# One fp32 mLSTM + MLP + four-expert kernel: GpSimd's order of weight pieces, and who prepares the input blocks of the second token half

## The reference, cut to what matters

```python
def _attn_ref(q, k, v, i_gate, f_gate, o_gate):   # (2, 8, 768, 40): a stabilized linear recurrence
    for t in range(S):
        C = f_stab * C + i_stab * outer(v_t, k_t);  n = f_stab * n + i_stab * k_t
        y_t = sigmoid(o_t) * (C q_t) / max(|n q_t|, 1)

def _moe_ref(x, w_in, w_out):                     # d_ff = 2048: "layer one" below
    h = x @ w_in
    return (h - np.tanh(h)) @ w_out

def _moe2_ref(x, domain_probs, w1, w2):           # 4 experts, 1024 hidden: "the experts" below
    p = domain_probs / (domain_probs.sum(-1, keepdims=True) + 1e-09)
    for e in range(4):
        out += p[:, e:e+1] * (np.maximum(x @ w1[e], 0.0) @ w2[e])
```

## Time and profile before

| what | us |
|---|---|
| median of 3 runs | 582.3 (580.66 to 582.67) |
| the profiled execution's own time | 584.62 |
| its span in the trace | 582.8 |
| PE busy | 567.1 (97%) |
| DVE, ACT, POOL busy | 346.7, 246.1, 245.3 |
| mean granted clock of TensorE | 0.991 of full speed |

### The profile page before, as it was taken

The page is one execution under the profiler, slowest core; times in us unless marked ns, Lnnn a source line. Parts: engine busy times, 40 slices in busy tenths (PEclk is TensorE's granted clock), DMA queues, the critical chain, the costliest instruction groups (busy, mean ns, idle before and its releaser), DMA issues.

```text
span 582.8 us, 10092 instructions
## 1 busy us (share of the span) xinstructions
PE 567.1 (97%) x3796; PEld 544.7 (93%) x3796; DVE 346.7 (59%) x663; ACT 246.1 (42%) x501; POOL 245.3 (42%) x238
## 2 busy tenths in 40 slices
PE   9999999999999999979999998999998999999997
PEld 8989999999998877869999998999998999999997
DVE  6656556555554486568754755645844646764644
ACT  5775645565534554524234432234522235422221
POOL 4878423333202677574006665026663046650000
PEclk9998999999999999989999999999998999999999
DMA  7977445654235021060002111002122002100201
GB/s 275 346 260 243 141 123 160 170 169 105 52 71 148 5 58 58 2 164 8 2 1 58 60 60 60 1 1 60 58 60 60 1 15 58 48 0 1 69 1 69
DMA packets 46359, 48.08 MB, mean 83 GB/s; under 512 B 21830, under 2 KB 36422, under 8 KB 46310
## 3 DMA queue, kind: packets, MB, share of 16 engines
q1 hardware_dynamic: 46208, 47.39, 27.2%
q10 hardware_dynamic: 102, 0.05, 0.0%
HBM read 41.12 MB, written 4.73 MB: 79 GB/s over the span
## 4 chain that ended last, share of the span: by engine, by line
PE 72%; POOL 11%; DMA 7%; DVE 3%; SPq 2%; issue 2%; ACT 1%; DVEq 0%; POOLq 0%; ACTq 0%
PE bank L1712 6%; PE bank L1713 6%; PE bank L1714 6%; DMA fast_raw<-in_w 5%; PE bank L1687 5%; PE bank L1690 5%; PE bank L1688 5%; PE bank L1689 5%; PE bank L1669 4%; PE bank L1670 3%; PE bank L1671 3%; PE bank L1640 3%; PE bank L1642 3%; PE bank L1641 3%; POOL fast_w L837 3%; POOL fast_w L829 2%
## 5 line engine op out<-in xcount | busy, mean ns | idle before, releaser
L1359 DVE TENSOR_TENSOR x<-bank,x 128x384 f32<-128x384 f32 x160 | 88.8, 555 | 75.6 <-PE bank L1690 73.6
L1712 PE MATMUL bank<-fast_w,g_tiles 128*128 128x320 f32 x384 | 119.8, 312 | 0.0
L1713 PE MATMUL bank<-fast_w,g_tiles 128*128 128x320 f32 x384 | 119.2, 310 | 0.0
L1714 PE MATMUL bank<-fast_w,g_tiles 128*128 128x320 f32 x384 | 119.1, 310 | 0.0
L1036 ACT ACTIVATE g_tiles<-x 128x384 fp32r<-128x384 f32 x96 | 50.4, 525 | 148.0 <-DVE x L1359 147.5
L1353 DVE SCALAR_TENSOR_TENSOR g_tiles<-x,g_tiles 128x384 fp32r<-128x384 f32 x96 | 69.7, 733 | 18.1 <-ACT g_tiles L1036 14.2
L1713 PEld LDWEIGHTS bank<-fast_w,g_tiles 128*128 128x128 f32 x384 | 73.1, 190 | 0.0
L1712 PEld LDWEIGHTS bank<-fast_w,g_tiles 128*128 128x128 f32 x384 | 72.9, 190 | 0.2 <-DVE arena L1301 0.2
L1714 PEld LDWEIGHTS bank<-fast_w,g_tiles 128*128 128x128 f32 x384 | 72.6, 189 | 0.0
L1306 DVE TENSOR_TENSOR bank<-bank,g_tmp 128x384 f32<-128x384 f32 (+2 forms) x64 | 36.1, 565 | 54.5 <-ACT g_tmp L991 54.1
L829 POOL TENSOR_TENSOR fast_w<-fast_raw,fast_w 128x512 fp32r<-128x512 f32 x16 | 21.7, 1356 | 96.0 <-ACT fast_w L977 95.9
(11 more groups left out here) (226 smaller groups left out, 1326.0 us busy)
## 6 DMA issues: line engine op xcount, KB each, us to landing
w_raw<-in_w SPq DMA_DIRECT2D x8, 704.0 KB, 7.3
zb<-z SPq DMA_DIRECT2D x10, 512.0 KB, 4.6
feat<-in_feat SPq DMA_DIRECT2D x10, 512.0 KB, 3.9
fast_raw<-in_w SPq DMA_DIRECT2D x16, 320.0 KB
tok<-in_tok SPq DMA_DIRECT2D x10, 484.0 KB, 4.6
fast_raw<-in_w SPq DMA_DIRECT2D x16, 256.0 KB
fast_raw<-in_w SPq DMA_DIRECT2D x32, 128.0 KB
spare<-xg SPq DMA_DIRECT2D x8, 256.0 KB, 2.8
```

The costliest lines, as they stand in the source:

```text
L1359: V.tensor_tensor(out, bank_of(u, name)[:, 0:WIDE], other, ALU.add).then_inc(summed, 1)
L1712: mm(out, g_tiles[:, k, 0, c], high_w, start=first, stop=False)
L1713: mm(out, g_tiles[:, k, 0, c], low_w, start=False, stop=False)
L1714: mm(out, g_tiles[:, k, 1, c], high_w, start=False, stop=stop).then_inc(third_done, 1)
```

## The change

1. Layer one's tables: `xa_low`, `xa_high`, `high_at` and `down_at` are shifted by a step in places; DVE casts a piece's second-layer weights before the low part of a block and not after it; ACT copies the first half of piece 3 in unit 0 of the experts and not in step 63.
2. POOL adds the x sums of the second half in two parts: the 256 main features before the tails have come, the tails after.
3. The blocks of the second half are made in later units (none in unit 1, five high parts in unit 2, two in unit 3), and POOL makes the low parts of T1 to T4; DVE keeps those of B11, B21 and B22. POOL does this ahead of the sums of piece 4. PE waits for each block apart.
4. For experts 1 to 3, POOL makes the low parts of pieces q and q+1 right behind each other, then the sums and the low parts of q+2, then those of q+3. Before, the sums of piece q+1 stood ahead of the low parts of piece q throughout. ACT copies the second-layer weights before the first-layer ones.

```diff
-        xa_high = {50: (B11,), 51: (B21,), 52: (B22,), 55: (T1, T2), 58: (T3, T4)}
-        xa_low = {53: B11, 54: B21, 55: B22, 56: T1, 57: T2, 59: T3, 60: T4}
-        high_at = {53: (0, 0), 54: (0, 1), 56: (1, 0), 57: (1, 1), 59: (2, 0), 60: (2, 1), 63: (3, 0)}
-        down_at = {54: 0, 56: 1, 60: 2, 62: 3}
+        xa_high = {50: (B11,), 51: (B21,), 52: (B22,), 55: (T1, T2), 59: (T3, T4)}
+        xa_low = {53: B11, 54: B21, 55: B22, 56: T1, 58: T2, 60: T3, 61: T4}
+        high_at = {53: (0, 0), 54: (0, 1), 57: (1, 0), 58: (1, 1), 60: (2, 0), 61: (2, 1)}
+        down_at = {53: 0, 57: 1, 60: 2, 63: 3}
...
+            def add_x_parts():
+                pool.wait_ge(x2_main, 8)
+                pool.wait_ge(block_ready, BLOCKS)
+                pool.wait_ge(xt_ready, len(L1_SIZES))
+                for i, one, two_ in x_parts(1):
+                    after(pool, x_main_sums, i - T1)
+                    G.tensor_tensor(x_sum(1, i)[:, 0, :], one[:, 0, :], two_[:, 0, :], ALU.subtract).then_inc(x_main_sums, 1)
+                pool.wait_ge(x_main_sums, 4)
+                pool.wait_ge(tails_in, 256)
+                for i, one, two_ in x_parts(1):
+                    after(pool, x_sums, 4 + i - T1)
+                    G.tensor_tensor(x_sum(1, i)[:, 1, :], one[:, 1, :], two_[:, 1, :], ALU.subtract).then_inc(x_sums, 1)
+
+            def x_block_low(i):
+                src, x = x_sum(1, i), x_block(1, i)
+                pool.wait_ge(block_high, BLOCKS + i + 1)
+                after(pool, late_ready, 2 * (i - T1))
+                G.tensor_tensor(x[:, 2, :], src[:, 0, :], x[:, 0, :].bitcast(F32), ALU.subtract).then_inc(late_ready, 1)
+                pool.wait_ge(late_ready, 2 * (i - T1) + 1)
+                G.tensor_tensor(x[64:KT, 1, :], src[64:KT, 1, :], x[64:KT, 1, :].bitcast(F32),
+                                ALU.subtract).then_inc(late_ready, 1)
...
-            add_x(1)
+            add_x_parts()
+            for i in (T1, T2, T3, T4):
+                x_block_low(i)
             pool.wait_ge(down_done, L1_STEPS)
-            add_weights(PPU)
-            for q in range(PPU, FAST):
-                if q + 1 < FAST:
-                    add_weights(q + 1)
+            for e in range(1, EXPERTS):
+                q = PPU * e
+                if e == 1:
+                    pool.wait_ge(late_ready, 8)
+                add_weights(q)
+                add_weights(q + 1)
                 low_weights(q)
+                low_weights(q + 1)
+                add_weights(q + 2)
+                low_weights(q + 2)
+                add_weights(q + 3)
+                low_weights(q + 3)
...
                 q = fast_at[u]
+                high_of_down(q)
                 high_weights(q, 0)
-                high_of_down(q)
...
                 if u == 0:
+                    high_weights(PPU - 1, 0)
                     evac(len(L1_SIZES) - 1)
...
-                if u == 2:
-                    x_block_high(1, B22)
-                if u == 3:
-                    x_block_high(1, T3)
+                for i in {2: (B11, B21), 3: (T3, T4)}.get(u, ()):
+                    x_block_high(1, i)
...
-                for i in {1: (B11, B21), 2: (T1, T2), 3: (T4,)}.get(u, ()):
-                    x_block_high(1, i)
+                if u == 2:
+                    for i in (B22, T1, T2):
+                        x_block_high(1, i)
...
-                if u in (1, 2, 3):
-                    x_block_low(1, {1: B11, 2: B22, 3: T3}[u])
+                if u == 3:
+                    x_block_low(1, B21)
```

More of the change, by code:

```diff
@@ L346, in mlstm_mlp_experts @@
         block_ready = sem("block_ready")
+        x_main_sums = sem("x_main_sums")
+        late_ready = sem("late_ready")
         fast_in = [sem(f"fast_in{r}") for r in range(FAST_RING)]
@@ L838, in low_weights, with x_parts @@
                                         w[:, F_DN:F_DN + 2 * D].bitcast(F32), ALU.subtract).then_inc(fast_down, 1)
[L840 to L850, removed]
+            def x_parts(h):
+                return ((T1, plain(h, -1), plain(h, B11)), (T2, plain(h, B22), x_sum(h, T1)),
+                        (T3, plain(h, B22), plain(h, -1)), (T4, plain(h, B21), x_sum(h, T2)))
@@ new lines, in add_x @@
+            def add_x():
+                pool.wait_ge(x2_main, 6)
+                pool.wait_ge(tails_in, 128)
+                for i, one, two_ in x_parts(0):
+                    after(pool, x_sums, i - T1)
+                    G.tensor_tensor(x_sum(0, i), one, two_, ALU.subtract).then_inc(x_sums, 1)
+            def add_x_parts():
[10 more added lines that the diff above has]
+                    G.tensor_tensor(x_sum(1, i)[:, 1, :], one[:, 1, :], two_[:, 1, :], ALU.subtract).then_inc(x_sums, 1)
@@ L852, in _ @@
             add_weights(0)
-            add_x(0)
+            add_x()
             for q in range(PPU):
@@ L1344, in _ @@
                     evac(m // L1_TILES - 1)
+                if m in down_at:
+                    high_of_down(down_at[m])
                 if m in xa_low:
                     x_block_low(0, xa_low[m])
-                if m in down_at:
-                    high_of_down(down_at[m])
             def low_tile(u, k, src):
@@ L1383, in _ @@
                     mix(v, TPH - 1)
-                if u in (2, 3, 4):
-                    x_block_low(1, {2: B21, 3: T2, 4: T4}[u])
                 low_tile(u, C11, bank_of(u, 2)[:, 0:WIDE])
@@ L1408, in _ @@
                 if u == 2:
-                    x_block_low(1, T1)
+                    x_block_low(1, B11)
+                if u == 3:
+                    x_block_low(1, B22)
             for tt in range(TPH):
@@ L1714, in third, with plain_block, sum_block @@
                 mm(out, g_tiles[:, k, 1, c], high_w, start=False, stop=stop).then_inc(third_done, 1)
-            def new_half(u, j):
-                if u % (2 * PPU) == PPU and u < 2 * PPU:
-                    pe.wait_ge(block_ready, BLOCKS + j + 1)
+            def plain_block(u, i):
+                if u == PPU:
+                    pe.wait_ge(block_ready, BLOCKS + i + 1)
+            def sum_block(u, i):
+                if u == PPU:
+                    pe.wait_ge(late_ready, 2 * (i - T1 + 1))
             for m in range(L1_STEPS):
@@ L1752, in _ @@
                     pe.wait_ge(fast_up, 2 * (4 * (u // (2 * PPU)) + u % PPU + 1))
-                new_half(u, B11)
+                plain_block(u, B11)
                 pe.wait_ge(summed, 5 * (u - 1) + (SUM_U2 if u == 1 else SUM_C21))
@@ L1757, in _ @@
                 third(u - 1, 1)
-                new_half(u, T2)
+                sum_block(u, T2)
                 if u > 1:
@@ L1764, in _ @@
                 third(u - 1, 3)
+                plain_block(u, B21)
                 pe.wait_ge(first_copied, u + 1)
@@ L1768, in _ @@
                 third(u - 1, 5)
-                new_half(u, T3)
+                sum_block(u, T3)
                 pe.wait_ge(summed, 5 * u + SUM_U2)
@@ L1777, in _ @@
                 third(u - 1, 9)
-                new_half(u, T4)
+                sum_block(u, T4)
                 pe.wait_ge(summed, 5 * u + SUM_U3)
@@ L1781, in _ @@
                 third(u - 1, 10)
+                plain_block(u, B22)
                 pe.wait_ge(summed, 5 * u + SUM_C22)
```

## The result

| | before | after |
|---|---|---|
| median of the runs of one session, us | 582.48 (580.66 to 584.56, 4 runs) | 574.01 (573.42 to 574.25, 4 runs) |
| ratio of the times, with its 95% interval | | 0.985 [0.982, 0.989] |
| the profiled execution, us | 584.62 | 573.42 |
| span, us; mean granted clock | 582.8; 0.991 | 571.6; 1.000 |
| PE busy, us | 567.1 (97%) | 563.1 (99%) |

The account below looks back on a forecast made before the run. PE was busy 567.1 of 582.8 us, so only its idle time and clock could be won. Terms 5.8 + 5.7 - 1.2 - 0.5 = 9.8 us off the median 582.3 gave 572.5 us; range 569 to 577.5.

Parts of the forecast that it names:

- Unit 1: Unit 1 of the experts: with no blocks there, PE's 4.1 us stop and 1.7 of clock go, 5.8 us off.
- half price for half an x sum: POOL's x sums, second half: half a sum takes half of 2.0, so 1.0 us; bounds 1.0 and 2.0.
- DVE's blocks in units 2 and 3: B11 at the end of unit 2 can collide with POOL's T3 and T4: 0 to 2.2 us, taken as 0.
- The two waits for POOL: PE's two 2.0 us waits for POOL's last low part of a piece go, with 1.7 of clock: 5.7 us.
- The new wait for C11: Units 9, 17 and 25: ACT's copy waits for POOL's sums and holds tile C11, 0.4 us each.
- with more room: Unit 9, on ACT: second high copy and tile C22 queue behind the late copy with more room; no cost added.
- The term "1.2": Units 9, 17 and 25: three waits of 0.4 us for tile C11, 1.2 us lost; bounds 0 and 2.4.
- Layer one: Layer one's waits for low parts: 2.7 us against 2.2, a loss of 0.5; bounds a gain of 1.6, a loss of 2.4.
- the 1 us that it gave as a sign: Layer one: waits of about 1 us after steps 53 and 60 would show the forecast holds.
- The 0.8 at step 57: Layer one, step 57: the wait from ACT, held by the sums of piece 1, goes, 0.8 us.
- The clock: PE's clock was to stand at 1.00 from 210 to 570 us; 1.7 us counted with each of two removed stalls.
- The rival in which the port takes the gain back: DVE loses at steps 53 and 60, C11 waits 0.8, one stall halves the clock: 5.0 us gained, 577.3; chance 0.15.

Follow-up runs that it names:

- part 4 alone: Kernel before plus only POOL's low parts of two pieces behind each other and ACT's second-layer copy first: 579.08 us, ratio 0.996.
- part 4 alone without ACT's swap: Kernel before plus only POOL's new order of pieces, ACT's first high copy still ahead of its second-layer copy: 576.56 us, ratio 0.991.
- part 1 alone: Kernel before plus only layer one's new tables, the cast ahead of the block and piece 3 copied in unit 0: 583.18 us, ratio 1.001.
- parts 2 and 3 alone: Kernel before plus only x sums in two parts, second-half blocks in later units and T1 to T4 low by POOL: 577.41 us, ratio 0.990.

## Why the prediction was right, point by point

- **Unit 1: right.** 5.8 forecast, 5.7 measured. From unit 1 to unit 5 the blocks alone give 5.1, as the whole change does. DVE's fifth sum waits for nothing but its product. The half price for half an x sum (1.0) was measured at 1.07 to 1.20.
- **DVE's blocks in units 2 and 3 at 0: off by 0.6**, inside the bounds of 0 to 2.2. B11 didn't collide, since POOL waited for T3's high part just then (row at 265.05). B21 in unit 3 did, with T4's low part, and unit 4 began 0.37 late; B22 did in unit 4, with the sums of piece 4 that now run there, and cost the other 0.20. That sums of weights would meet a block was in neither the term nor its bounds.
- **The two waits for POOL: right.** 5.7 forecast, 5.8 measured. Piece 7's low parts end at 337.9, PE begins unit 11 at 346.8: 8.9 us to spare, 7.5 forecast.
- **The new wait for C11: the mechanism right, the term too small.** Sums of piece 7 were forecast to end at 337.8 on the clock of before, and C11 to be ready at 339.95; measured, with 7.9 added, 337.8 and 340.0, and a wait of 0.40 in the list where 0.4 was forecast (0.56 by the starts). The step that failed is the sentence that the second high copy and tile C22 are queued behind it "with more room". I counted room for ACT, not the port: the late tile moved C22 behind the start of a POOL instruction. The term "1.2" measured 3.5 when its cause alone was taken away, and 3.2 against before, which had lost 0.3 in units 17 and 25 itself. Beside it stands 1.0 that nobody forecast: units 7, 15 and 23 and the ones next to them are 0.1 to 0.25 shorter than before. The net is the 2.2 of the table; part of the size of the sum is luck by that.
- **Layer one: the size right, the way not quite.** 0.5 forecast, 0.7 measured by the starts, and 0.76 with the tables alone. I put 1.0 on each of steps 53 and 60, in the middle between a DVE that wins and one that loses the tie. It won at step 53 (row at 197.46). What it cost there was 0.20. PE stood longer one step on (0.54), since the block instructions of step 54 were stretched as well (1.21 and 1.27), and at 221.69 (0.38) behind block T2, moved to step 58 by the tables (1.56 and 1.27). Step 60's pair cost 0.27 and step 61's 0.52; the forecast named only the pairs of steps 53 and 60. No wait reached the 1 us that it gave as a sign. So the sum came out near by errors that offset each other. The 0.8 at step 57 did go.
- **The clock: right.** 1.00 from layer one to the end; behind none of the waits that were left (0.5 us at most there) did it fall in this trace.
- The rival in which the port takes the gain back had the right mechanism for the 1.8 us that are missing, but not the places: C22 in units 9, 17 and 25, not C11, and the blocks in units 3 and 4.
- The profiled execution of before was 2.1 us above its median, and its trace had the wait of 1.3 and the 3.4 us of half clock in the attention stage that the trace of after had not. Subtracting terms from the median, as the prediction did, kept that out. Whoever subtracts the two spans reads 11.2 us, and 3.2 of it lie outside the change.

## What to carry to other kernels

- Cost a late instruction by what it collides with when it is late, not only by how late it is: here 0.4 us on one tile cost 1.15 us a unit. Where an engine waits for another in a copy that nobody needs soon, put the copy behind the work that is due (3.5 us by the traces for one copy moved).
- Where DVE and GpSimd both read SBUF, compare start times of both engines to some hundredths of a us; an edit that shifts GpSimd by 0.3 to 0.8 us moved this kernel by 2 to 3 us, once in either direction, so try both orders and keep the measured one. And undo parts of a change that has won: the tables of layer one only cost (43.5 us from step 53 to unit 0 in the traces with them, 42.7 to 42.8 without).
- Line up two traces by the same matmul in each stage before giving a difference of spans to a change, and price a wait by the starts of matmuls around it, not by the list of waits alone.

## What the runs showed of the hardware

- **The same idle time cost 3.4 us of half clock, or 6.8.** Windows around the end of the wait of 4.0 in unit 1 (the number behind the engines is the granted clock), of before and of part 4 alone:

```profile
256.00:270.00 14.00, 11.48 (x61) 11.12 (x62) 12.25 (x15) 4.78 (x9) 12.47 (x11) 0.88 0.30 91
```

```profile
250.00:270.00 20.00, 16.04 (x84) 15.78 (x83) 14.02 (x18) 7.32 (x12) 14.61 (x12) 0.83 0.31 90
```

  The clock was at 1.2 GHz, half, for 14.00 x 0.12 / 0.5 = 3.4 us and for 20.00 x 0.17 / 0.5 = 6.8 us. With part 4 alone without ACT's swap, and with part 1 alone, it was 6.8 too (0.83 over 20 us). After a wait of 2.0 for POOL it fell or not: before, only after the second; with parts 2 and 3 alone, only after the first (0.83 from 351 to 361, 1.00 from 430 to 440). With part 1 alone, too, only after the first (two waits of 2.4). What decides it stays open; these traces show about the same idle time with both outcomes.
- **Who is first decides, down to some hundredths of a us.** I take every pair, in all fourteen traces from 190 us on, of a DVE instruction with both inputs in SBUF (the block instructions and the low parts of tiles) and a POOL `TENSOR_TENSOR` that overlaps its first 0.55 us. Where DVE started first, 93 times, and 18 of them by only 0.03, DVE took 0.54 to 0.56. Where POOL started first and had over 0.06 left, 631 times, and once by only 0.01, DVE ended 0.41 to 0.48 after POOL's end: POOL to 335.56 and DVE to 335.97 in the change. So a stretched DVE instruction is priced as what is left of POOL's and 0.42 more.
- **The stretch works both ways:** POOL's 640 columns took 1.57 when it was first and 1.77 to 1.78 when DVE was (rows of unit 9 above).
